# Six of eight blank blocks written by GpSimd, and another order of SyncE's first loads

## The chip, the core and the metric

The kernel runs on one core of one Trainium2 chip. The metric is the device time of the whole program in microseconds. All engines of the core (TensorE, VectorE, ScalarE, GpSimd, SyncE) and its 16 DMA engines are the kernel's own.

## The reference

Three stages follow one another, all in float32. Attention over 4 x 8 heads with 576 tokens of 64 dimensions, with a causal mask by blocks of 64; a dense layer with softplus; a layer with eight experts, one per token, which only computes tokens with a positive skip score.

```python
scores = where(block_i >= block_j, q @ k.T / 8, -1e9)
attn = exp(scores - max) ; attn = attn / (sum(attn) + 1e-9)
x = (attn @ v), heads side by side              # 2304 tokens x 512
h = x @ w_in                                    # 512 x 2048
x = (max(h, 0) + log1p(exp(-abs(h)))) @ w_out   # 2048 x 512
out = x
xc = x[x @ w_skip > 0]                          # the tokens that are computed
probs = softmax(xc @ w_gate) ; e = argmax       # 8 experts
out[those] = xc + probs[e] * (max(xc @ w1[e], 0) @ w2[e])
```

## The kernel before

Every engine has a program of its own, written out by hand in an order that is fixed when the kernel is built; they meet by semaphores. An engine takes its instructions in order, and a wait holds up all that stands behind it on that engine.

**Attention.** The 32 heads are worked in 16 pairs. TensorE turns queries and keys (`turn_qk`, L336 to 346), makes five row blocks of scores per pair (`score`, L367 to 398), and in the next pair's step turns the probabilities (`turn_probs`, L414 to 424) and mixes the values (`mix_left`, L426; `mix_right`, L442). VectorE takes the maxima and copies some of the turned tiles, ScalarE takes the exponents and copies the others, GpSimd scales the probabilities and splits the weights of the dense layer into two parts (`split`). A turned tile lies in one of two banks in turn, so a turn waits for the copy of the tile two before it (`bank_free`, L329). The first step differs from the later ones: pair 0's queries and keys come in two halves.

SyncE issues the loads (`sync`, L211 to 289). `load_qk(p)` is six DMAs for one pair: two of queries with 128 KB each, one of 32 KB for the last 64 rows, and the same for keys; for p = 2 or 3 it waits for the turning of the ends of pair p - 2, whose buffers it fills. `load_v(p)` is three DMAs, and waits from p = 2 on. `load_weights(w)` is one DMA of 512 KB. Ahead of the loop stand `load_first_q`, `load_qk(1)`, a wait for VectorE's zeros, `load_v(0)`, `load_v(1)` and `load_weights(0)` (L264 to 269); the loop's step p then issues `load_qk(p + 2)` and the rest.

**Dense layer.** Six blocks of 384 tokens, 16 columns of the hidden layer each. After each block its tokens are routed, and GpSimd scatters their rows to `x_sorted` in DRAM (`sort`, L1123), which has a region for each expert.

**Experts.** Tokens are worked in tiles of 64 rows. Tiles that are full after five of the six blocks are "early" and are read while the last block is routed; they number three in these inputs, and four later ones follow. A region's last tile can run past its rows. So, when the last block's places are known, 64 blank rows (128.5 KB, with a target that is out of bounds) are written behind the rows of each of the eight experts: `close` (L978 to 983). SyncE closes the first `E - CLOSED_BY_POOL` experts after its store of the last rows (L1051), GpSimd the others right after the last `sort` (L1138). Each needs its address from a table, read into a register of the issuing engine (`entry`, L966). SyncE then waits for the table of the later tiles, the sorted rows and both counts of closed experts (L1054 to 1057), and loads the first two later tiles (L1058 to 1061). VectorE copies the first (`copy_x`, L1781), and TensorE turns it (`turn_x`, L1280) in the middle of the last early tile. GpSimd's queue goes on with the stores of the results (`store_tile`, L1140), for which VectorE waits two tiles later (`finish`, L1787).

Of the kernel before, what the change touches and what calls it, by code (L numbers as in the profile page):

```python
# [67 lines left out]
def build(nc, q, k, v, w_in, w_out, w_skip, w_gate, w1, w2, out):  # L68
# [31 lines left out]
    with whole:  # L100
        ident = sb(whole, "ident", [P, P])
        with ExitStack() as feed:

            win = {p: sb(feed, f"w_in_{p}", [P, DM // P, FF], F32R) for p in ("high", "low")}
            wout = {p: sb(feed, f"w_out_{p}", [P, FF // P, DM], F32R) for p in ("high", "low")}
            x_raw = sb(feed, "x_raw", [P, DM // P, TILES * P])
            router = sb(feed, "router", [P, DM // P, GROUP])
            x_stored = sem("x_stored")
            attended = attention(nc, qf, kf, vf, w_in, w_out, w_gate, w_skip, x_heads, ident, win, wout, x_raw, router,
                                 x_stored, sem, sb, ps, (B, H, S, D, PAIRS, JP, CH, FULL, TAIL, SCALE, DM, FF, E))  # L110
            rest(nc, x_heads, x_sorted, out, w_out, w1, w2, ident, win, wout, x_raw, router,
                 x_stored, PAIRS, attended, feed, sem, sb, ps, (N, DM, FF, E, EF))


def attention(nc, qf, kf, vf, w_in, w_out, w_gate, w_skip, x_heads, ident, win, wout, x_raw, router,
              x_stored, sem, sb, ps, sizes):
    B, H, S, D, PAIRS, JP, CH, FULL, TAIL, SCALE, DM, FF, E = sizes
    own = ExitStack()
    with own:
# [67 lines left out]
        def turned_count(step, name):  # L187
            return units[step, name] + 1
# [5 lines left out]
        def ends_counted(p):  # L194

            return min(p, PAIRS - 1) - 1
# [14 lines left out]
        def sync(sp):  # L211
            def load_first_q():

                for half in range(2):
                    c = slice(2 * half, 2 * half + 2)
                    for two in range(2):
                        sp.dma_start(q_nat[:, 0, c, two, :],
                                     qf[two, 2 * half * P:(2 * half + 2) * P, :].rearrange("(c p) d -> p c d", p=P))\
                          .then_inc(q_loaded[0] if half else s["first_half_loaded"], 16)
                for nat, src in ((q_nat, qf), (k_nat, kf)):  # L220
                    sp.dma_start(nat[0:TAIL, 0, FULL, :, :], src[0:2, FULL * P:S, :].rearrange("a p d -> p a d"))\
                      .then_inc(ends_loaded[0], 16)

            def load_qk(p):
                if p in (2, 3):
                    sp.wait_ge(s["turned_ready"], turned_count(p - 3, "ends"))
                if p > 3:
                    sp.wait_ge(s["ends_turned"], ends_counted(p - 2))
                for nat, src, loaded in ((q_nat, qf, q_loaded), (k_nat, kf, k_loaded)):
                    for two in range(2):  # L230
                        sp.dma_start(nat[:, p % 2, 0:FULL, two, :],
                                     src[2 * p + two, 0:FULL * P, :].rearrange("(c p) d -> p c d", p=P))\
                          .then_inc(loaded[p % 2], 16)
                    sp.dma_start(nat[0:TAIL, p % 2, FULL, :, :],
                                 src[2 * p:2 * p + 2, FULL * P:S, :].rearrange("a p d -> p a d")).then_inc(ends_loaded[p % 2], 16)

            def load_v(p):
                if p > 1:
                    sp.wait_ge(s["mixed_right_ready"], p - 1)
                for two in range(2):  # L240
                    sp.dma_start(v_nat[:, p % 2, two, 0:FULL, :],
                                 vf[2 * p + two, 0:FULL * P, :].rearrange("(c p) d -> p c d", p=P))\
                      .then_inc(v_loaded[p % 2], 16)
                sp.dma_start(v_nat[0:TAIL, p % 2, :, FULL, :],
                             vf[2 * p:2 * p + 2, FULL * P:S, :].rearrange("a p d -> p a d")).then_inc(v_loaded[p % 2], 16)

            def load_weights(w):
                b = w % 2
                if w > 1:
                    sp.wait_ge(s["weights_split"], w - 1)  # L250
                if w < 8:
                    sp.dma_start(stage[:, b, :], w_in[(w // 2) * P:(w // 2 + 1) * P, b * HALF:(b + 1) * HALF])\
                      .then_inc(w_loaded[b], 16)
                else:
                    f = 2 * (w - 8)
                    sp.dma_start(stage[:, b, :].rearrange("p (f n) -> p f n", n=DM),
                                 w_out[f * P:(f + 2) * P, :].rearrange("(f p) n -> p f n", p=P)).then_inc(w_loaded[b], 16)

            def store(p):
                sp.wait_ge(s["mixed_right_copied"], p + 1)  # L260
                sp.dma_start(x_heads[(p % JP) * P:(p % JP + 1) * P, (p // JP) * S:(p // JP + 1) * S], x_pair[:, :])\
                  .then_inc(x_stored, 16)

            load_first_q()  # L264
            load_qk(1)
            sp.wait_ge(s["zeros_ready"], 1)
            load_v(0)
            load_v(1)
            load_weights(0)
            for p in range(PAIRS + 2):  # L270

                if p < PAIRS - 2:
                    load_qk(p + 2)
                if 1 < p < PAIRS:
                    load_v(p)
                if 0 < p < LAST_PART:
                    load_weights(p)
                if p > 1:
                    store(p - 2)
                if p == JP + 1:  # L280
                    assert TILES * P <= S
                    sp.wait_ge(x_stored, 16 * JP)
                    sp.dma_start(x_raw[:], x_heads[:, 0:TILES * P].rearrange("(k p) t -> p k t", p=P))\
                      .then_inc(s["first_loaded"], 16)
                    with nc.allow_non_contiguous_dma(reason="512 values, once"):
                        sp.dma_start(router[:, :, 0:E], w_gate.rearrange("(k p) e -> p k e", p=P))\
                          .then_inc(s["first_loaded"], 16)
                        sp.dma_start(router[:, :, E:E + 1], w_skip.rearrange("(k p o) -> p k o", p=P, o=1))\
                          .then_inc(s["first_loaded"], 16)
# [378 lines left out]
        def vector(dve, split_x):  # L668
# [133 lines left out]
            return copies_late  # L802

    return sync, gpsimd, tensor, scalar, vector, s, turned_count


def rest(nc, x_heads, x_sorted, out, w_out, w1, w2, ident, win, wout, x_raw, router,
# [149 lines left out]
    with late:  # L957
# [20 lines left out]
        def close(engine, queue, experts, closed):  # L978

            engine.wait_ge(s["tally_ready"], 2)  # L980
            for e in experts:
                queue.dma_start(x_sorted[bass.ds(entry(engine, FIRST_FREE, e, E * EACH - ROUND), ROUND), :], empty[:])\
                    .then_inc(s[closed], 16)

        CLOSED_BY_POOL = 3

        block = late.enter_context(nc.Block())

# [1 line left out]
        def _(sp):  # L990
# [59 lines left out]

            close(sp, sp, range(E - CLOSED_BY_POOL), "closed")  # L1051


            sp.wait_ge(s["tally_ready"], 3)  # L1054
            sp.wait_ge(s["sorted"], 16 * TILES * BLOCKS)
            sp.wait_ge(s["closed"], 16 * (E - CLOSED_BY_POOL))
            sp.wait_ge(s["closed_by_pool"], 16 * CLOSED_BY_POOL)
            for number in range(AHEAD):  # L1058
# [27 lines left out]
        def _(pool):  # L1086
# [50 lines left out]

            close(pool, nc.gpsimd, range(E - CLOSED_BY_POOL, E), "closed_by_pool")  # L1138

# [722 lines left out]
```

## Time and profile before

| | |
|---|---|
| three runs | 683.88, 684.08, 687.5 us; median 684.08 |
| the profiled execution | 684.91 us |
| its span, first to last instruction | 683.2 us |
| TensorE busy | 669.7 us, 98% of the span |
| VectorE, ScalarE, GpSimd busy | 432.6, 403.2, 166.1 us |
| granted TensorE clock, mean | 0.998 of full |
| moved by DMA | 53.73 MB |

The page gives the busy time of each engine, the share of each engine in the chain of work that ended last, and groups of instructions by line. "SPq" and "POOLq" are the sequencers of SyncE and GpSimd: they load registers, wait and issue, and count as busy in no sum.

### The profile page before, as it was taken

The page shows a single profiled execution, that of the slowest core. Times are in us where ns is not written, and L with a number is a line of the kernel's source. Part 1 is how long each engine was busy: PE and PEld are TensorE (multiplying, and loading weights), DVE is VectorE, ACT ScalarE, POOL GpSimd, SP SyncE. Part 2 cuts the span into 40 slices and gives each one's busy share as a digit, 9 for nine tenths or more (in the row PEclk, how much of TensorE's full clock was granted, in tenths as well). Part 3 has the DMA queues.
Part 4 walks back from the last instruction along what each step waited for, and adds up shares of the span by engine and source line. Part 5 has one row for each costly group of instructions (what it writes and reads, how often), then busy time and mean ns, then how long its engine had stood idle before and what let it go on. Part 6 is the DMA issues. An engine that isn't in the chain of part 4 may idle for free.

```text
span 683.2 us, 12963 instructions
## 1 busy us (share of the span) xinstructions
PE 669.7 (98%) x3982; PEld 519.1 (76%) x3982; DVE 432.6 (63%) x1048; ACT 403.2 (59%) x993; POOL 166.1 (24%) x228
## 2 busy tenths in 40 slices
PE   7999999999999999999999999999999999999995
PEld 5666656566689999889988998989889988874442
DVE  6767676767756676577657765776567656845222
ACT  5676767666865666566665665566656665542221
POOL 3776767676830000010001000010002000202111
PEclk9999999999999999999999999999999999999999
DMA  7656765654130002000200011000200010069270
GB/s 168 168 142 160 187 164 136 165 136 132 36 112 2 1 0 94 1 10 1 69 23 2 7 39 53 0 0 3 89 0 13 1 46 0 11 248 367 73 266 19
DMA packets 79471, 53.73 MB, mean 79 GB/s; under 512 B 61256, under 2 KB 64328, under 8 KB 79424
## 3 DMA queue, kind: packets, MB, share of 16 engines
q1 hardware_dynamic: 76048, 50.50, 25.4%
q0 software_dynamic: 1968, 1.86, 1.0%
q10 hardware_dynamic: 1408, 0.79, 0.4%
q8 instruction: 24, 0.39, 0.2%
q14 instruction: 23, 0.19, 0.1%
HBM read 41.18 MB, written 16.28 MB: 84 GB/s over the span
## 4 chain that ended last, share of the span: by engine, by line
PE 89%; DVE 4%; SPq 3%; issue 2%; DMA 1%; ACT 0%; POOL 0%; DVEq 0%; POOLq 0%; ACTq 0%
PE hidden L1177 10%; PE hidden L1179 9%; PE hidden L1178 9%; PE rows_out L1190 9%; PE rows_out L1188 9%; PE rows_out L1189 9%; PE turned L423 7%; PE scores L390 6%; PE mixed L451 5%; PE hidden L1293 3%; PE rows_out L1308 3%; PE scores L396 2%; PE turned L344 2%; PE mixed L438 2%; PE turned_y L1217 1%
## 5 line engine op out<-in xcount | busy, mean ns | idle before, releaser
L1406 ACT ACTIVATE mag<-hidden 128x384 f32<-128x384 f32 x96 | 47.1, 491 | 151.3 <-PE hidden L1179 151.3
L1177 PE MATMUL hidden<-x_parts,w_in_high 128*128 (+1 forms) x384 | 132.8, 346 | 0.4 <-DVEq L1600 0.4
L1179 PE MATMUL hidden<-x_parts,w_in_low 128*128 (+1 forms) x384 | 129.5, 337 | 0.0
L1178 PE MATMUL hidden<-x_parts,w_in_high 128*128 (+1 forms) x384 | 129.4, 337 | 0.0
L1127 POOL DMA_INDIRECT x_sorted<-y,slot x18 | 20.2, 1120 | 402.2 <-DVE slot L1649 398.6
L1190 PE MATMUL rows_out<-w_out_high,g_low 128*128 128x512 f32 x288 | 114.2, 396 | 0.0
L1188 PE MATMUL rows_out<-w_out_high,g_high 128*128 128x512 f32 x288 | 113.7, 395 | 0.4 <-DVE g_low L1607 0.4
L1189 PE MATMUL rows_out<-w_out_low,g_high 128*128 128x512 f32 x288 | 113.5, 394 | 0.0
L299 POOL TENSOR_SCALAR probs<-probs,inverse 128x128 f32<-128x128 f32 (+3 forms) x128 | 67.4, 545 | 55.8 <-DVE inverse L703 55.8
L1607 DVE TENSOR_TENSOR g_low<-g,g_high 128x384 fp32r<-128x384 f32 x96 | 54.7, 570 | 37.3 <-DVE g L1598 35.0
L1177 PEld LDWEIGHTS hidden<-x_parts,w_in_high 128*128 128x128 f32 x384 | 72.2, 188 | 8.1 <-issue 3.1
L560 ACT ACTIVATE probs<-scores,neg_max 128x128 f32<-128x128 f32 (+3 forms) x126 | 65.3, 528 | 21.2 <-DVE neg_max L691 11.6
L1178 PEld LDWEIGHTS hidden<-x_parts,w_in_high 128*128 128x128 f32 x384 | 72.3, 188 | 2.1
L1179 PEld LDWEIGHTS hidden<-x_parts,w_in_low 128*128 128x128 f32 x384 | 72.1, 188 | 0.0
L1592 DVE TENSOR_SCALAR small<-u 128x384 uint32<-128x384 f32 x96 | 34.7, 361 | 56.7 <-ACT u L1408 55.6
L1597 DVE COPY_PREDICATED log<-small,series 128x384 f32<-128x384 uint32 x96 | 58.7, 611 | 17.3 <-DVE series L1594 17.3
L1190 PEld LDWEIGHTS rows_out<-w_out_high,g_low 128*128 128x128 f32 x288 | 54.1, 188 | 12.5
L1188 PEld LDWEIGHTS rows_out<-w_out_high,g_high 128*128 128x128 f32 x288 | 54.1, 188 | 9.4 <-DVE g_low L1607 1.1
L1189 PEld LDWEIGHTS rows_out<-w_out_low,g_high 128*128 128x128 f32 x288 | 54.1, 188 | 8.7
L1594 DVE SCALAR_TENSOR_TENSOR series<-square,u 128x384 f32<-128x384 f32 x96 | 53.3, 555 | 4.5
L1598 DVE SCALAR_TENSOR_TENSOR g<-hidden,log 128x384 f32<-128x384 f32 x96 | 53.5, 557 | 3.3
L1410 ACT ACTIVATE square<-u 128x384 f32<-128x384 f32 x96 | 50.6, 527 | 3.0
(209 smaller groups left out, 1036.8 us busy)
## 6 DMA issues: line engine op xcount, KB each, us to landing
whole_w<-in_moe_w_dram SPq DMA_DIRECT2D x12, 1024.0 KB, 11.3
x_heads<-x_pair SPq DMA_DIRECT2D x16, 288.0 KB, 4.7
x_raw<-x_heads SPq DMA_DIRECT2D x6, 768.0 KB, 5.6
out_dram<-y SPq DMA_DIRECT2D x6, 768.0 KB, 4.0
v_nat<-in_v_dram SPq DMA_DIRECT2D x32, 128.0 KB, 2.4
stage<-in_moe_w_in_dram SPq DMA_DIRECT2D x8, 512.0 KB, 4.5
q_nat<-in_q_dram SPq DMA_DIRECT2D x30, 128.0 KB, 2.6
k_nat<-in_k_dram SPq DMA_DIRECT2D x30, 128.0 KB, 2.6
```

What stands on the lines that cost most here:

```text
L299: nc.gpsimd.tensor_scalar(to, to, inverse[:, i, two:two + 1], 1.0, ALU.mult, ALU.mult)\
L560: last = nc.scalar.activation(to, scored, ACT.Exp, bias=neg_max[:, i, two:two + 1], accum_out=sums[:, i, two:two + 1])
L1177: nc.tensor.matmul(o, win["high"][:, k, cols], high, start=(k == 0), stop=False)
L1178: nc.tensor.matmul(o, win["high"][:, k, cols], low, start=False, stop=False)
L1179: last = nc.tensor.matmul(o, win["low"][:, k, cols], high, start=False, stop=(k == K - 1))
L1188: nc.tensor.matmul(o, high, wout["high"][:, f, :], start=(f == 0), stop=False)
L1189: nc.tensor.matmul(o, high, wout["low"][:, f, :], start=False, stop=False)
L1190: return nc.tensor.matmul(o, low, wout["high"][:, f, :], start=False, stop=(f == F - 1))
L1594: step.then(nc.vector.scalar_tensor_tensor(series[:], square[:, b, :], REST, u[:, b, :], ALU.add, ALU.mult))
L1597: step.then(nc.vector.copy_predicated(log[:, b, :], small[:], series[:]))
L1598: step.then(nc.vector.scalar_tensor_tensor(g[:, b, :], hidden[:, b, 0:T], 0.0, log[:, b, :], ALU.max, ALU.add))
L1607: nc.vector.tensor_tensor(g_low[f % RING][:], g[:, f % 2, :], g_high[f % RING][:], ALU.subtract)\
```

## The change

`load_weights(0)` and pair 2's six loads of queries and keys stand ahead of the wait for the zeros and of the six loads of values for pairs 0 and 1; the loop's step 0 issues nothing in exchange. `CLOSED_BY_POOL` is 6, so SyncE closes experts 0 and 1, GpSimd 2 to 7.

```diff
             load_first_q()
             load_qk(1)
+            load_weights(0)
+            load_qk(2)
             sp.wait_ge(s["zeros_ready"], 1)
             load_v(0)
             load_v(1)
-            load_weights(0)
             for p in range(PAIRS + 2):
 
-                if p < PAIRS - 2:
+                if 0 < p < PAIRS - 2:
                     load_qk(p + 2)
...
-        CLOSED_BY_POOL = 3
+        CLOSED_BY_POOL = 6
```

## Rows read from the trace of the kernel before

**Rows 1.** The page: span, and the engines' shares of the chain that ended last.

```profile
span 683.2 us, 12963 instructions
...
PE 89%; DVE 4%; SPq 3%; issue 2%; DMA 1%; ACT 0%; POOL 0%; DVEq 0%; POOLq 0%; ACTq 0%
```

**Rows 2.** Windows: length, then each engine's busy time, granted clock, DMA share, GB/s.

```profile
0.00:195.00 195.00, 191.08 (x1417) 121.10 (x1418) 132.60 (x335) 135.71 (x417) 130.35 (x180) 1.00 0.55 141
600.00:684.00 84.00, 74.06 (x470) 38.13 (x468) 27.83 (x84) 20.25 (x50) 11.15 (x13) 0.98 0.58 196
```

**Rows 3.** Timeline of SyncE's queue at the start: start us, us, what is issued.

```profile
8.11 1.14 SPq L241 DMA_DIRECT2D v_nat<-in_v_dram  x2
...
11.79 0.59 SPq L252 DMA_DIRECT2D stage<-in_moe_w_in_dram  x1
12.43 0.99 SPq L231 DMA_DIRECT2D q_nat<-in_q_dram  x2
...
15.95 1.14 SPq L231 DMA_DIRECT2D q_nat<-in_q_dram  x2
```

**Rows 4.** The chain in order of time, at pair 2's queries: start us, us.

```profile
12.90 3.33 DMA q_nat<-in_q_dram
```

**Rows 5.** Timeline of TensorE at the start; in brackets idle time before, and releaser.

```profile
6.71 0.22 PE L357 MATMUL turned<-ident,q_nat 64*128 64x64 f32 x1
...
16.27 0.66 PE L344 MATMUL turned<-ident,q_nat 128*128 128x128 f32 x4 [0.52 <-DMA q_nat<-in_q_dram]
...
17.19 1.13 PE L390 MATMUL scores<-kT,qT 64*128 64x512 f32 x4
...
19.27 0.87 PE L438 MATMUL mixed<-probsT,v_nat 128*64 128x256 f32 x8
```

**Rows 6.** Timeline of SyncE's queue at the end: its blank blocks.

```profile
625.61 6.22 SPq L982 DMA_DIRECT2D x_sorted<-shared  x5
```

**Rows 7.** The chain in order of time, from SyncE's last blank block on.

```profile
631.35 3.69 DMA x_sorted<-shared
...
635.90 2.63 DMA softplus_done<-x_sorted
```

**Rows 8.** Timeline of TensorE at the first later tile.

```profile
639.33 0.43 PE L1285 MATMUL tile_x_turned<-ident,other_x 64*128 64x64 f32 x4 [0.88 <-DVE other_x L1785]
```

**Rows 9.** Timeline of ScalarE at the start: a copy from a bank, an accumulator read.

```profile
15.79 0.48 ACT L569 COPY probsT<-turned 128x384 f32<-128x384 f32 x1
...
16.54 0.20 ACT L560 ACTIVATION_READ_ACCUMULATOR probs<-scores,neg_max 128x1 f32 x1
```

**Rows 10.** Timeline of VectorE: the table of later tiles, the third early tile's result.

```profile
631.77 0.17 DVE L1769 CAST tiles<-shared 1x32 int32<-1x32 f32 x1
...
641.92 0.74 DVE L1795 SCALAR_TENSOR_TENSOR mag<-rows_out,other_x 64x512 f32<-64x512 f32 x1 [2.51 <-PE rows_out L1308]
```

**Rows 11.** Timeline of GpSimd at the end.

```profile
628.82 1.64 POOL L982 DMA_DIRECT2D x_sorted<-shared  x3
631.69 0.95 POOL L1143 DMA_INDIRECT out_dram<-yT,first_result_to  x1 [1.24 <-issue]
```

**Rows 12.** Line 982 on GpSimd: ns min/median/max, first and last start; landing of all three.

```profile
L982 POOLq MOVE x_sorted<-shared x3: 29/29/29, 626.9 to 629.2; - x3
...
DMA to landing us min/median/max: 3.4/4.2/4.6
```

**Rows 13.** Line 1143 between 634 and 636 us: MOVE and DMA of one store.

```profile
L1143 POOLq MOVE  x1: 29/29/29, 634.3 to 634.3; - x1
L1143 POOL DMA_INDIRECT out_dram<-x_raw,result_to x1: 933/933/933, 635.1 to 635.1; - x1
```

**Rows 14.** Line 1135: one blank block that GpSimd writes alone at 586.6.

```profile
DMA to landing us min/median/max: 3.0/3.0/3.0
```

**Rows 15.** Windows around the blank blocks, columns as in rows 2.

```profile
629.00:631.00 2.00, 2.00 (x12) 0.76 (x14) 1.79 (x7) 0.74 (x2) 1.45 (x3) 1.00 0.98 274
...
633.00:635.00 2.00, 2.00 (x20) 1.14 (x16) 1.02 (x2) 0.38 (x1) 0.00 (x0) 1.00 0.60 151
```

## The prediction

> **What bounds the kernel now.** I read the page first, then the windows by stage, then the two places that the diff touches. The page's chain says TensorE for 89% of the span, the DMA queues for a few per cent [rows 1]. By stage TensorE is busy 191.08 of the first 195 us, and 74.06 of the last 84 [rows 2]: what idle time it has lies at the very start and in the expert stage at the end. The diff works at just these two ends. In the 400 us between them nothing that it edits runs.
>
> At the start the chain runs through SyncE's issues: SyncE hands out loads one after another, the two value loads of pairs 0 and 1 ahead of the weights and of pair 2's queries [rows 3]; the queries are issued last, land 3.33 us after their issue [rows 4], and TensorE has been idle for 0.52 us when it turns them at 16.27 [rows 5].
>
> At the end the chain leaves TensorE when the last place table is ready: SyncE issues five blocks of blank rows one by one from 625.61, 6.22 us of them [rows 6], the fifth at 631.35 lands 3.69 us later, at 635.04, and only then do the first later rows go out at 635.90, land after 2.63 us [rows 7] and reach TensorE. Its idle time there is 0.88 us [rows 8]. It is so short because TensorE still has the third early tile to do.
>
> **The start, step by step.** In the new order the weights (0.59 us of issue, with the gap 0.64) go first, at 8.11, and pair 2's six loads follow at 8.75. These six take 15.95 - 12.43 = 3.52 us of SyncE [rows 3], so the values start at 12.27 and not at 8.11, and pair 3's queries at 15.95 as before: nothing is added or removed, the order alone changes. The wait of pair 2's loads is for the turning of pair 0's ends, at 6.71 [rows 5], before these loads are reached, and the wait for zeros has long been met, so neither holds up the queue.
> - Gain. The second query load is issued some 3.7 us earlier and lands by about 9.2 + 3.3 = 12.5, before 15.75 (16.27 - 0.52), when TensorE wants it. What is late next? The second turn of probabilities needs the bank that ScalarE empties from 15.79 to 16.27, and the scores after it need ScalarE's exponent, whose accumulator read ends at 16.54 + 0.20 = 16.74 [rows 9]. These scores start at 17.19 now [rows 5]. With the bank free at about 16.33 and the same 0.53 us from the turn to the scores they start at 16.86. The gain is 17.19 - 16.86 = 0.33 us, with bounds 0 and 0.52; I take 0.35. TensorE has no free time in the pairs that follow, so it is kept to the end.
> - Price. Pair 0's values are now issued from 12.27, their last at some 13.5. The value loads are no larger than the query load that landed 3.33 us after its issue [rows 4]: by 16.8. They are wanted at 19.27 [rows 5], 18.9 after the gain. The cover is 2.1 us; past it each us costs a us. Cost 0.
>
> **The end, step by step.** SyncE keeps two blocks: it is done at about 628 and not 631.83, and then stands at the table (ready at 631.77 + 0.17 = 631.94 [rows 10]) and at GpSimd's blocks. So GpSimd's last block alone decides.
> - GpSimd's issues now: it starts three blocks from 628.82 in 1.64 us, 0.55 each [rows 11]. Read so, the sixth would start at 628.82 + 5 x 0.55 = 631.6. But these three ran back to back only because they had queued up behind the sorting of the last rows. The registers for each are loaded by GpSimd's sequencer, and its three MOVEs stand from 626.9 to 629.2, so 1.15 us apart [rows 12]. That is the pace of a fourth, fifth and sixth: MOVEs at 630.35, 631.5 and 632.65. A MOVE at 634.3 had its DMA start at 635.1, 0.8 us after [rows 13]; the sixth block so starts at about 633.45.
> - From start to landing: 3.0 us for a block alone [rows 14]; 3.4, 4.2 and 4.6 for the three that shared the DMA engines with the weights, SyncE's blocks and each other [rows 12]. The engines are full between 629 and 631 (0.98) and at 0.60 between 633 and 635 [rows 15]. In the new kernel the last three blocks come 1.15 us apart, with SyncE's two long in front: I take 3.2, nearest to the lone row. Bounds 3.0 and 4.6.
> - Sum: the sixth lands at 633.45 + 3.2 = 636.65 against 635.04, so 1.6 us later. The later rows, the copy on VectorE and TensorE's turn follow at the same distance; TensorE's idle time grows from 0.88 to about 2.5 us and nothing after it can take it back, since the chain from there on is TensorE's tiles.
> - Behind the blocks on GpSimd stand the stores of the first results: the first (631.69 [rows 11]) moves by three MOVEs, to about 635.1, the second from 635.1 to about 636.1, landing by 640. VectorE needs both before the third tile's result, formed at 641.92 now [rows 10] and 1.6 later then. Hidden by more than 1.9 us.
>
> The Trainium skill, "DMA: Bandwidth & Descriptors", section "Anatomy of one DMA", fits a GpSimd DMA by 2.0 us and its bytes at 436 GB/s: an estimate of 2.3 us for 128.5 KB. The lone block here took 3.0 [rows 14], so the trace differs; by the page the end would lose 0.7 us and the whole 0.35.
>
> **Sum.** -0.35 at the start, +1.6 at the end: +1.25 us. The profiled execution took 684.91 us (span 683.2), so 686.2 by its own time; it was 0.83 above the median of the three runs, 684.08, and the forecast for the median is 685.3.
>
> **Rivals.**
> 1. GpSimd issues the blocks back to back (0.55 us). The sixth starts at 631.6 and lands after 3.0 to 3.4: 634.6 to 635.0, the end gains 0 to 0.4. With the start: 683.3 to 683.7. For it: three blocks that did run so; against it: their MOVEs.
> 2. The DMA engines' backlog, not the issue, sets the last landing. All eight blocks are the same bytes for the same 16 engines, which were full until about 634 [rows 15]; then the last of them lands at about 635.0 as before, and only the start counts: 683.7. Against it: a block issued at 633.45 can't be part of a backlog that ends at 634, so this needs rival 1's pace too. The Trainium skill, the same page, section "Issuing engines are not separate DMA queues", says just this: spreading DMAs over engines saves only the time of the sequencers. [rows 12] say that here the sequencer loses some.
> 3. Landing grows with each block in GpSimd's queue, as 3.4, 4.2, 4.6 [rows 12]: 0.6 more each gives 6.4 for the sixth. It lands at 639.85, 4.8 us late; net +4.45, 688.5, which is slower by over 0.5%. It decides from a landing time of 5.4 us on. Against it: the growth was seen while five of SyncE's blocks and the weights used the same engines; they are gone. A milder form, 4.6 for the last, lands at 638.05: +3.0, net +2.65, 686.7.
> 4. The values are late for the first mix (over 2.1 us beyond the worst landing seen). Against: no load in these rows took over 3.33 us. It would cost the excess; I give it no number above 1 us.
>
> **Chances.** Forecast 0.62; rivals 1 and 2 together 0.2; the mild form of rival 3 0.1, its full form 0.04; the rest, rival 4 and other things, 0.04. 0.5% is 3.4 us, about what a measurement of this kernel can tell from no change. Only the full form of rival 3 reaches it, and no case gains over 1.3 us (0.35 and all of TensorE's 0.88): faster 0.02, same 0.93, slower 0.05. The range runs from rival 1 to a little above the mild form of rival 3 and has to hold the spread of the runs (683.88 to 687.5): 683.4 to 687.3.
>
> **What the changed profile would show.** At the start: no idle time of TensorE before pair 2's queries; the scores behind at 16.9; the first mix without a wait for values. At the end: GpSimd's L982 MOVEs still 1.15 us apart, its last block starting at 633.1 (all of it 0.35 earlier than written above) and landing at 636.3; SyncE's wait ended by GpSimd's count and not its own; TensorE's idle time before the first later tile at 2.5 us. I am wrong if the six blocks run at 0.55 us each, if the last of them lands before 635 or after 638, or if the mix waits for values.

## The result and the profile after

The changed kernel is slower: 687.78 us median of 7 runs (686.58 to 689.55) against 684.98 (683.88 to 687.5, 7 runs), a ratio of 1.004 with a 95% interval of 1.003 to 1.005. That is 2.8 us. It lies above my range (683.4 to 687.3), though within the 0.5% for which I gave 0.93. The profiled execution took 687.05 us, 2.14 more than the profiled one of before.

| | before | after |
|---|---|---|
| profiled execution, span | 684.91, 683.2 us | 687.05, 685.4 us |
| TensorE busy | 669.7 us | 671.6 us |
| mean granted clock | 0.998 | 0.995 |
| last blank block lands | 635.04 | 636.07 |
| TensorE's wait at the first later tile | 0.88 us | 1.85 us |

**The start**, as rows 5 had it: the timeline of TensorE in the changed kernel (start us, us; in brackets the idle time before).

```profile
5.32 0.66 PE L411 MATMUL mixed<-ident,q_nat 128*128 128x128 f32 x2 [0.23 <-DMA k_nat<-in_k_dram]
...
7.24 0.22 PE L358 MATMUL turned<-ident,q_nat 64*128 64x64 f32 x1
...
16.35 0.63 PE L345 MATMUL turned<-ident,q_nat 128*128 128x128 f32 x4
...
17.41 1.13 PE L391 MATMUL scores<-kT,qT 64*128 64x512 f32 x4
...
19.49 0.87 PE L439 MATMUL mixed<-probsT,v_nat 128*64 128x256 f32 x8
```

The wait for pair 2's queries is gone and no wait for values has come. Yet the ends of pair 0 are turned at 7.24 and not at 6.71 [rows 5]: the kernel is 0.53 us late before any reordered load matters, and 0.22 us late (17.41 against 17.19) behind the reordered loads. So the new order gave 0.31 us, and something else took 0.53. That stretch, from the turning of pair 0's ends to these scores, takes 10.16 to 10.20 us in all nine profiles with the new order (here and below), and 10.21 to 11.28 us in the eight with the old one: the new order takes away a wait whose length varies, from nothing to 1.1 us. The two turnings at 5.32 took 0.66 us; the same two of before are in the next fence, 0.41 us. The fence's two lines of GpSimd are marks: the first store of the last block's sorting, and the last store of a result.

```profile
5.39 0.41 PE L410 MATMUL mixed<-ident,q_nat 128*128 128x128 f32 x2 [0.16 <-DMA k_nat<-in_k_dram]
...
625.16 1.11 POOL L1127 DMA_INDIRECT x_sorted<-y,slot  x1 [37.97 <-DVE slot L1649]
...
678.92 0.91 POOL L1143 DMA_INDIRECT out_dram<-x_raw,result_to  x1 [8.28 <-DVE x_raw L1799]
```

Both executions begin with turnings of 0.59 to 0.69 us for two; this one keeps that pace longer. It looks like the array's clock rising later, but the clock column says 1.00 in both for these microseconds, so this is read from durations only.

**The end**: the timeline of GpSimd, which answers to rows 11 (its first and last line are the same two marks), and line 983 there, which answers to rows 12.

```profile
625.28 1.11 POOL L1128 DMA_INDIRECT x_sorted<-y,slot  x1 [37.97 <-DVE slot L1650]
...
628.94 1.64 POOL L983 DMA_DIRECT2D x_sorted<-shared  x3
631.08 0.53 POOL L983 DMA_DIRECT2D x_sorted<-shared  x1 [0.50 <-issue]
632.47 0.52 POOL L983 DMA_DIRECT2D x_sorted<-shared  x1 [0.86 <-issue]
633.61 0.52 POOL L983 DMA_DIRECT2D x_sorted<-shared  x1 [0.62 <-issue]
635.19 0.95 POOL L1144 DMA_INDIRECT out_dram<-yT,first_result_to  x1 [1.06 <-DVE x_raw L1800]
...
681.36 0.91 POOL L1144 DMA_INDIRECT out_dram<-x_raw,result_to  x1 [8.28 <-DVE x_raw L1800]
```

```profile
L983 POOLq MOVE x_sorted<-shared x6: 29/29/29, 627.0 to 633.1; - x6
...
DMA to landing us min/median/max: 2.5/3.0/3.1
```

Three blocks start back to back, then one at a time with idle time "issue" between them: that is the sequencer's pace, (633.1 - 627.0) / 5 = 1.22 us a MOVE. Taken one by one, the six land after 2.9, 3.1, 3.1, 3.0, 2.7 and 2.5 us. The chain in order of time, for rows 7, and TensorE's timeline, for rows 8:

```profile
633.61 2.46 DMA x_sorted<-shared
...
636.88 2.74 DMA softplus_done<-x_sorted
```

```profile
640.42 0.43 PE L1286 MATMUL tile_x_turned<-ident,other_x 64*128 64x64 f32 x4 [1.85 <-DVE other_x L1786]
```

Now the windows behind that wait (length, then each engine's busy time, granted clock, DMA share, GB/s), first of the changed kernel, then of the one before.

```profile
640.00:646.00 6.00, 5.58 (x30) 2.70 (x32) 1.91 (x4) 0.37 (x1) 0.00 (x0) 0.72 0.09 27
```

```profile
640.00:646.00 6.00, 6.00 (x44) 3.14 (x42) 1.91 (x3) 1.05 (x4) 0.96 (x1) 1.00 0.08 24
```

The granted clock is 0.72 over these six microseconds. At its lower level, 1.2 GHz, it is 0.5, so it lay there for 6 x 0.28 / 0.5 = 3.4 us. Behind the last 0.42 us of its wait TensorE is busy without a gap, and yet the window holds 30 products where it held 44 before. This is what the prediction did not have. The 2.14 us split at marks that both profiles have:

| stretch | before | after | difference |
|---|---|---|---|
| to the last block's sorting on GpSimd | 625.16 | 625.28 | +0.12 |
| to TensorE's first later tile | 14.17 | 15.14 | +0.97 |
| to GpSimd's last store | 39.59 | 40.94 | +1.35 |
| to the end of the execution | 5.99 | 5.69 | -0.30 |

The second line is the wait, the third the clock: the same instructions on the same data, the four later tiles. The table explains the 2.14 us between the two profiled executions. The medians are 2.8 us apart, since the profiled executions lie 0.07 us (before) and 0.73 us (after) below theirs; where that 0.7 us lies no profile shows.

### The profile page after: what moved, and what is told of

The parts are those of the page before. It is cut to its first block, busy times and chain, and to the rows that moved or that the text cites. A ratio compares the mean times of both kernels' runs of the same rounds, so it can differ in the third digit from the quotient of the medians.

```text
span 685.4 us, 12963 instructions
## 1 busy us (share of the span) xinstructions
PE 671.6 (98%) x3982; PEld 519.9 (76%) x3982; DVE 432.7 (63%) x1048; ACT 403.6 (59%) x993; POOL 168.0 (25%) x231
## 4 chain that ended last, share of the span: by engine, by line
PE 90%; DVE 5%; issue 2%; DMA 1%; POOLq 1%; POOL 0%; ACT 0%; ACTq 0%; DVEq 0%; SPq 0%
PE hidden L1178 10%; PE hidden L1180 9%; PE hidden L1179 9%; PE rows_out L1191 9%; PE rows_out L1189 9%; PE rows_out L1190 9%; PE turned L424 7%; PE scores L391 6%; PE mixed L452 5%; PE rows_out L1309 3%; PE hidden L1294 3%; PE scores L397 2%; PE turned L345 2%; PE mixed L439 2%; PE turned_y L1218 1%
```

## The experiments

They ran on four chips, those of one set together, each set against runs of the kernel before on the same chip. "Clock theory" is what the last table says; its rivals are that each part of the change costs by issue alone, and that the loads' new order costs. A figure recurs below: the mean granted clock of each timed run. It has the last microseconds, in which TensorE has ended, in it; a fall of 3.4 us takes 3.4 x 0.5 / 685 = 0.0025 off it. I count a run as fallen at 0.995 or below. The seventeen profiled executions bear this out: the five with a fall behind the wait have 0.993 to 0.995, the twelve without one 0.996 to 0.999. But the mean doesn't say where in a run the clock was low, so for a run without a profile "fallen" is inferred.

"The mark" below is the start of GpSimd's first store of the last block's sorting (625.16 before, 625.28 after). The last blank block lands 9.88 us behind it before, 10.79 after.

**First set: each part by itself, and the wait filled.**

```diff
# e1_order: the changed kernel with
-        CLOSED_BY_POOL = 6
+        CLOSED_BY_POOL = 3
# e2_pool6, e3_pool4: the kernel before with 6, with 4
# e4_pool6_fill: e2 and, in tile(), for every early tile of the second expert
+                for _ in range(fill):      # 8
+                    nc.tensor.matmul(turned_y[:, 0:P], ident[:], ident[:], start=True, stop=True)
                 if late:
                     turn_x(turn + 1)
```

> The new order of SyncE's loads alone, GpSimd at three blocks. Clock theory (the loss is TensorE's longer idle time at the end and the drop of its clock behind it; the order is worth -0.3 us): the end as before with 0.9 us of idle time and no drop, time -0.6 to +0.3 us against before, the spread from when the clock rises at the start. Order theory (the loss comes from the loads): +1 us or more, with a wait in the first pairs. Either way pair 2's queries are turned without a wait for their load.

Measured: 685.78 us against 685.77, ratio 0.9998 (0.9988 to 1.0009). No loss from the order, so the order theory falls. A gain of 0.3 us is inside the interval (-0.8 to +0.6 us) and not shown by it. In its profile pair 2's queries are turned without a wait; in e2's, with the old order on the same chip, TensorE waited:

```profile
17.01 0.66 PE L344 MATMUL turned<-ident,q_nat 128*128 128x128 f32 x4 [1.31 <-DMA q_nat<-in_q_dram]
```

> GpSimd writes six blocks, the loads in their old order. Clock theory: the last block starts at 633.5 and lands near 636, TensorE idles 1.9 us, its clock falls to 1.2 GHz for some 3.4 us after that, time +2.5 to +3.2 us against before. If the issue alone costs: +1.0 us with the clock at full. Order theory: +1 us or less.

Measured: 687.09 us, ratio 1.0021 (1.0011 to 1.003), so +1.4 us. The wait was 1.63 us in the profile, without a fall; 3 of the 12 timed runs were fallen (687.94 to 688.88 us; the others 686.32 to 687.45). The median is neither theory's number, but the two groups are: the nine other runs have a median of 686.78, +1.0 us against before, as foretold for issue alone, and the three fallen ones 688.61, +2.8, as foretold with the clock.

> GpSimd writes four blocks, SyncE four. By the issue times in the two profiles SyncE's fourth starts at 630.1 and GpSimd's fourth at 631.1 and lands at 634.1, so the later rows come 0.9 us sooner and TensorE has 0 to 0.2 us of idle time there: -0.7 to -0.9 us against before. Rival (the DMA engines' backlog sets the last landing whoever issues): 635.0 as before and no change.

Measured: 685.87 us, ratio 0.9993 (0.9984 to 1.0003): no gain is shown, though the interval doesn't exclude one. GpSimd's fourth block took 4.63 us to land, and the DMA engines were still full between 632 and 634:

```profile
632.00 4.63 DMA x_sorted<-shared
```

```profile
632.00:634.00 2.00, 2.00 (x13) 0.79 (x14) 1.04 (x5) 0.37 (x1) 0.53 (x1) 1.00 0.98 218
```

It landed 10.39 us behind the mark; with three blocks on GpSimd, on the same chip (e1), the last one landed after 10.28. So the last landing came no sooner though the last issue did, as the rival says: with four the DMA engines' backlog sets it. The third set asks what that backlog is.

> Six blocks by GpSimd as in the run with that alone, and eight matrix products of the identity with itself (results unused) put on TensorE where it waits for the first later rows: some 1.7 us of work in an idle time of 1.9 us. Clock theory: the rows come as late as without them, the clock stays at 2.4 GHz, and the time is 1.5 to 1.7 us below that run, +1.0 us against before. If the wait alone costs: no change against that run, or a little slower.

Measured: 689.37 us, ratio 1.0049 (1.0036 to 1.0063). A flaw of the experiment: the second expert has two early tiles, so 16 products ran and not 8, those of the first in no wait at all. That adds some 2 us (8 x 0.256), which is about what it is above e2 (2.3). No fall in its six runs, but it tells nothing of the price.

**Second set: longer waits, and one of them filled in the right tile only.** f1_after is the changed kernel. f2_pool8 and f4_pool1 are the kernel before with 8 and 1. f3_pool8_fill is f2 with the filling of e4, 14 products, in the last early tile alone:

```diff
-                    with pe.Fori(0, of_second) as j:
-                        tile(of_first + j, of_first + j, 1, late=True)
+                    tile(of_first, of_first, 1, late=True)
+                    with pe.If(of_second > 1):
+                        with pe.Fori(1, of_second) as j:
+                            tile(of_first + j, of_first + j, 1, late=True, fill=14)
```

> The changed kernel once more, beside the others on one chip. Clock theory: if TensorE's idle time before the first later tile is near 1.85 us or above, the clock falls behind it and the time is +2.5 to +3 us; if it is near 1.6 us, as in the run with six blocks alone, no drop and +1.0 to +1.5 us. Issue theory (each step costs by itself, the clock plays no part): +1.3 us whatever the idle time.

Measured: 687.67 us against 685.78, ratio 1.0031 (1.0019 to 1.0042); wait 2.01 us; fallen in 6 of 6 runs. The fall came as the clock theory had it, but the loss, +1.9 to +2.1 us, lies between the two theories' numbers.

> GpSimd writes all eight blocks, loads in the old order. Two more blocks at 1.15 to 1.4 us each: the last lands 2.3 to 2.8 us later than with six, TensorE idles about 4.2 us. Clock theory: the clock then falls to 1.2 GHz for 3 us or more, so +5.0 to +6.0 us against before. Issue theory: +3.7 to +4.0 us, clock at full.

Measured: 691.2 us, ratio 1.0082 (1.007 to 1.0095), +5.4 us: as the clock theory had it. The wait was 4.54 us, and then the clock was low for nearly seven microseconds:

```profile
643.60 0.66 PE L1285 MATMUL tile_x_turned<-ident,other_x 64*128 64x64 f32 x4 [4.54 <-DVE other_x L1785]
```

```profile
643.00:646.00 3.00, 2.40 (x10) 1.08 (x12) 0.56 (x2) 0.37 (x1) 0.00 (x0) 0.51 0.12 40
646.00:650.00 4.00, 4.00 (x18) 1.81 (x16) 1.49 (x2) 0.00 (x0) 0.00 (x0) 0.51 0.12 33
```

> All eight blocks by GpSimd, and 14 products of the identity with itself on TensorE in the last early tile alone, where it waits: 14 x 0.256 = 3.6 us of work in an idle time of about 4.2 us. Clock theory: the rows come as late, the clock stays at 2.4 GHz, and the time is 1.5 to 1.7 us below the run without the products. Issue theory: the same time as that run.

Measured: 688.92 us, ratio 1.0046 (1.0034 to 1.0058). That is 2.3 us less than f2 with 14 products more (1.5 to 1.7 were foretold), and none of its six runs was fallen, where all six of f2 were. The rows account for little of it: TensorE turns the first later tile at 644.01, 17.47 us behind the mark, against 17.86 in f2, and the stretch from there to the last store is 2.87 us shorter. So the time lost behind the wait is the clock's, at eight blocks. f3 also has its loop peeled, and there is no run of eight blocks with the peeling alone. The fence has two records for each product.

```profile
639.75 3.39 PE L1347 MATMUL turned_y<-ident 128*128 128x128 f32 x28
...
644.01 0.43 PE L1285 MATMUL tile_x_turned<-ident,other_x 64*128 64x64 f32 x4 [0.87 <-DVE other_x L1789]
```

```profile
643.00:646.00 3.00, 2.13 (x14) 0.81 (x12) 0.56 (x2) 0.37 (x1) 0.00 (x0) 1.00 0.14 44
```

> SyncE writes seven blocks, GpSimd one. SyncE's pace is 1.35 us a block, so its seventh starts 2.7 us after its fifth did and lands some 2 us later than before (it no longer meets a backlog): TensorE idles 2.5 to 3 us. Clock theory: the clock falls here too, though GpSimd has less to do: +3.3 to +4 us against before. If it is GpSimd's own queue (the stores behind its blocks) that costs: +1.9 us or less.

Measured: 688.53 us, ratio 1.0042 (1.0026 to 1.0058), +2.9 us, between the two theories' numbers; wait 2.41 us, fallen in 5 of 6 runs. GpSimd writes one block here, so its stores behind the blocks are not what costs. Any late last block does.

**Third set: fewer bytes in front of the blocks.** SyncE's 768 KB store of the last rows goes behind its loads of the later rows.

```diff
-            store_rows(BLOCKS - 1)
             close(sp, sp, range(E - CLOSED_BY_POOL), "closed")
...
                   .then_inc(c["later_x_loaded" if number else "later_first_loaded"], 16)
+            store_rows(BLOCKS - 1)
```

> The kernel before (SyncE five blocks, GpSimd three), with SyncE's 768 KB store of the last rows moved from ahead of its blank blocks to behind its loads of the first two later tiles. Backlog theory (with three or four blocks on GpSimd the last landing is set by the queue of bytes at the DMA engines): these bytes are gone from the front, the last block lands 1.5 to 2.5 us sooner, TensorE has no idle time there, -0.9 us. Issue theory (SyncE's fifth block, issued at 631.4, sets it): it still needs some 3 us, lands at 634.3, -0.7 us. Both give a gain; the landing time tells them apart.

Measured: 686.03 us against 685.7, ratio 0.9999 (0.999 to 1.0008). No gain, where both theories had one. SyncE's fifth block still took 3.99 us to land, 9.31 us behind the mark: 0.6 us sooner than in the first profile of before, not 1.5 to 2.5. With the store gone the DMA engines are full all the same, with little moved (206 GB/s) while the blank blocks are under way:

```profile
632.00:634.00 2.00, 2.00 (x16) 0.92 (x14) 1.46 (x6) 0.00 (x0) 0.95 (x1) 1.00 0.98 206
```

So the 768 KB are not what fills the engines at the end; that the blank blocks themselves do is likely, and not shown. The wait was 0.61 us, and 0.45 us of idle time came up in front of the next tile's products. The profile names no releaser for it. All four kernels of this set have it (0.36 to 0.61 us) and no other kernel has; its cause is open.

> The same with the new order of the first loads, GpSimd still at three blocks: -1.2 us, the sum of -0.9 and -0.3.

Measured: 685.06 us, ratio 0.9989 (0.998 to 0.9998). It beats the kernel before on this chip, by 0.6 to 0.7 us, with an interval that barely clears it. Against g1 (1.0 us by the medians, 0.3 foretold) the new order of the loads is the only difference, and in g1's profile TensorE had waited 0.99 us for pair 2's queries.

> The changed kernel (GpSimd six blocks) with the store moved as well. If GpSimd's issuing sets the last landing, it stays at 635.9 to 636.1, though the DMA engines have less to do, TensorE idles 1.6 to 2 us and the clock may fall: +1.0 to +2.8 us against before. If it was the DMA engines, the landing comes some 2 us sooner and the time is that of the run with three blocks, -1.2 us.

Measured: 687.36 us, ratio 1.0028 (1.0017 to 1.004). The chain has GpSimd's sixth block as in the changed kernel:

```profile
633.27 3.00 DMA x_sorted<-shared
```

It lands at 636.27, 11.22 us behind the mark, though 768 KB less stood in front. With six the issue sets the landing. The wait was 2.33 us; the profiled run kept its clock, six of the seven runs were fallen.

> Store moved, new order, GpSimd four blocks and SyncE four: both issuers are done at 630.1 and 631.1, so the last landing is not above 634.1 and may be near 633.5. TensorE is busy until 638.4 and needs the landing by 634.2; no gain over three blocks that a timing could show: -1.2 us.

Measured: 685.03 us, ratio 0.9991 (0.9981 to 1.0001): as g2.

**Fourth set: the clock's part in the changed kernel itself.** h3_after is the changed kernel; h2_after_peeled has the peeled loop of f3 and no products; h1_after_fill has seven of them.

> The changed kernel on the same chip as the two others: +2.0 us against before, between the two earlier timings of it (+2.1 by 1.0031 and +2.8).

Measured: 685.97 us against 685.42, ratio 1.0004 (0.9993 to 1.0016). The expected +2.0 us did not come: on this chip the changed kernel loses next to nothing. Its wait was 1.56 us, and its twelve runs fall into two groups: nine between 685.5 and 686.62 us (median 685.84, clock 0.998 or 0.999) and three at 687.44 to 687.95 (clock 0.995, 0.995 and 0.996). The profiled run is of the second:

```profile
640.84 0.43 PE L1286 MATMUL tile_x_turned<-ident,other_x 64*128 64x64 f32 x4 [1.56 <-DVE other_x L1786]
```

```profile
640.00:643.00 3.00, 2.16 (x10) 1.01 (x12) 0.57 (x2) 0.37 (x1) 0.00 (x0) 0.76 0.15 44
643.00:646.00 3.00, 3.00 (x18) 1.34 (x16) 0.99 (x2) 0.00 (x0) 0.00 (x0) 0.67 0.13 32
```

One program on one chip, with 1.6 us between the groups' medians (687.45 - 685.84): +0.4 and +2.0 us against before.

> The same code with no product filled in, so only the loop around that tile is peeled: the time of the changed kernel within 0.4 us, +2.0 us against before, with the clock falling.

Measured: 686.57 us, ratio 1.0012 (0.9999 to 1.0025); no run fallen. Its wait was 0.86 us, because TensorE came to it later, and for this reason:

```profile
630.47 0.41 PE L1303 MATMUL rows_out<-ident,x_raw 128*128 128x128 f32 x2 [1.44 <-ACT x_raw L1511]
```

h3 has 0.74 us of idle time at this place. So has h1, with the same peeled loop, and so it isn't shown that the peeling made it 1.44.

> The changed kernel with seven products of the identity with itself (7 x 0.256 = 1.8 us) on TensorE in the last early tile, where it waits some 1.9 us. Clock theory: landing and first later tile at the same times, clock at 2.4 GHz throughout, 1.3 us less than without the products (the difference that the profiles show from the first later tile to the last store, 39.6 against 40.9 us): +0.7 to +1.1 us against before. If the clock costs nothing: +2.0 us, as without them.

Measured: 688.82 us, ratio 1.0047 (1.0029 to 1.0066). The expectation failed. Six runs were fallen (689.54 to 691.17 us), six were not (686.31 to 688.1). In the profiled run, one without a fall, the products fitted the wait: without them TensorE would have stood from 638.84 to 641.15, for 2.3 us, and 0.56 us of it were left. Why the clock fell in half of the runs although the wait was filled, when it fell in none of h2's, and why that cost over 3 us, is open. So the filling shows the clock's price at eight blocks only; in the changed kernel itself it failed, and the price rests on the two groups of h3 and on the profiles.

**The waits and the clock together.** From TensorE's first later tile to GpSimd's last store, both from the profiled runs:

| kernel | wait, us | clock behind it | first later tile to last store, us | timed runs fallen |
|---|---|---|---|---|
| e4 (filled) | none | full | 39.26 | 0 of 6 |
| h1 (filled) | 0.56 | full | 39.75 | 6 of 12 |
| e3, e1 | 0.57, 0.58 | full | 39.57, 39.59 | 0 of 24 |
| g1, g4, g2 | 0.61, 0.63, 0.69 | full | 39.92, 40.08, 39.88 | 0 of 33 |
| h2 | 0.86 | full | 39.47 | 0 of 12 |
| f3 (filled) | 0.87 | full | 39.51 | 0 of 6 |
| before | 0.88 | full | 39.59 | 6 of 98 |
| h3 | 1.56 | fell | 40.94 | 2 of 12 (3 by their times) |
| e2 | 1.63 | full | 39.48 | 3 of 12 |
| after, f1 | 1.85, 2.01 | fell | 40.94, 40.89 | 13 of 13 |
| g3 | 2.33 | full | 40.04 | 6 of 7 |
| f4 | 2.41 | fell | 40.94 | 5 of 6 |
| f2 | 4.54 | fell, twice as long | 42.38 | 6 of 6 |

The stretch takes some 39.5 us at full clock and 1.35 more with one fall, whoever wrote the blocks. The extra 0.3 to 0.6 of the g kernels is the idle time in front of the next tile, 0.58 us in g3. The longer the wait, the more often the clock falls, with h1 as the exception; it is no switch, since 1.56 us had a fall in its profile, 1.63 and 2.33 none. Each wait is that of one profiled execution.

The waits of the same six blocks, 1.56 to 2.33 us, depend on when the rows come and also on when TensorE comes to the wait. In the profiles of before, after, f1 and g3 TensorE is done with what stands ahead of the wait 13.3 us behind the mark; in e2 and h3 after 14.1 us, since it had idled for 0.80 and 0.74 us shortly before 630.05 and 629.39 us. The profile names no releaser for that idle time. The rows did not come sooner in those two: the first later tile is turned 15.76 and 15.63 us behind the mark, against 15.14 in after and 15.29 in f1. So the shorter waits of e2 and h3 stand beside later rows and not earlier ones.

## Why the prediction was wrong

- **The new order of the loads: right.** 0.35 us foretold, 0.31 between 7.24 and 17.41. That it is so near is partly luck: against the other profiles of the old order the same stretch gains from nothing to 1.1 us. No wait for values, as priced. The start as a whole lost 0.12 all the same, by the slower turnings of its first microseconds; I had no term for how these differ from one execution to the next.
- **GpSimd's pace: right.** MOVEs at 627.0 to 633.1 us, the sixth block at 633.61, where I had 633.45. Two errors stand against each other in that: the sixth MOVE came at 633.1 and not 632.65, and the block started 0.5 us behind it and not 0.8. This was the choice between two readings of the same rows (0.55 us from the blocks, 1.15 from the MOVEs), and rival 1 falls.
- **The landing: too dear.** I took 3.2 us from start to landing with bounds 3.0 and 4.6; it was 2.46, below the lower one. To this landing the estimate of 2.3 us from the Trainium skill ("DMA: Bandwidth & Descriptors", "Anatomy of one DMA") was nearer than the lone block of rows 14; in the other profiles of six blocks the last took 2.63 (f1), 2.89 (h3), 2.96 (e2) and 3.00 us (g3), nearer to that block. With six blocks the latency doesn't grow along the queue but falls, from 3.1 to 2.5 us, so rival 3 falls too. The wait became 1.85 us, not 2.5. Rival 2 (the backlog) holds for four blocks (e3) and not for six (g3).
- **The stores behind the blocks: right**, hidden.
- **The step that failed** is the sentence "TensorE's idle time grows from 0.88 to about 2.5 us and nothing after it can take it back, since the chain from there on is TensorE's tiles". I priced the longer wait at its own length and took what follows as fixed. Just because the chain is TensorE's tiles there, it is open to TensorE's clock: the fall to 1.2 GHz for 3.4 us cost 1.35 us in the profiles, more than the wait itself (0.97). I named no rival for it. With that term the landing as foretold would have given 684.98 - 0.35 + 1.6 + 1.35 = 687.6.
- **The base** was low as well. I added +1.25 to 684.08, the median of three runs; seven give 684.98. From there the same range would have reached 688.2 and held the result. As a difference the result is +2.8 against +1.25, more than twice the forecast; of that the profiles give 1.35 us to the clock.

The size of the whole differs between the chips: +2.8 us in the first timing, +1.9 by the medians of f1, +0.55 on the chip of h3, where the clock fell in a quarter of the runs.

## What to carry to other kernels

Price a wait of TensorE in front of dense work as two terms, its length and the clock behind it, and give the second a chance that grows with the length; here it came in 3 of 12 runs or fewer at 1.6 us and in 13 of 13 at 1.85 to 2.0. When work moves to another issuer, count that issuer's registers per DMA and not only its DMAs; and ask whether issue or backlog sets the last landing, since only then does moving issues help. Here the last blank block landed 9.9 to 10.4 us behind the mark with three or four of the eight on GpSimd and the store in its place, 10.8 to 11.4 with six or with one, and over 13 with eight: a lopsided split is later to either side.

## What was not expected of the hardware

- The clock fell behind waits as short as 1.56 us, in some executions of a program and not in others; a fall lasted 3.4 us, but nearly 7 at the wait of 4.54 us.
- Filling the wait kept the clock up with eight blocks (no run of 6 fallen, against 6 of 6), and didn't with six (h1, 6 of 12).
- The kernel before has a mean clock of 0.995 or below in 6 of 98 timed runs, all six among its slow ones (686.99 us and more). Its wait is 0.88 us in the one profile; that these runs had the same fall, and at this place, is inferred.
- A block of 128.5 KB from GpSimd lands in 2.46 us when the DMA engines are little used (0.34 between 634 and 636 us) and in 4.63 when they are full (0.98 between 632 and 634 us in e3).
